# Splitting the attention output: the subtraction moves from the Pool engine to VectorE, and an unrounded copy goes

## The reference, cut to what matters

```
out[chunk] = softmax(q_c @ k_full.T / 8) @ v_full        # 64 keys for 32 queries
x = out as (3072 tokens, 512)
h = x @ w_in                                             # 512 -> 2048
x = (h * sigmoid(h)) @ w_out                             # 2048 -> 512
e = argmax(x @ w_gate + modality_bias[modality_id])      # one of 8 experts
y = gate * (relu(x @ w1[e]) @ w2[e])                     # 512 -> 1024 -> 512
```

## Time and profile before

| | |
|---|---|
| Median of 3 runs | 1037.0 us (1035.72 to 1037.22) |
| The profiled execution, its own time | 1038.32 us |
| Its span, first to last instruction | 1036.7 us |
| TensorE (PE) matmuls busy | 976.9 us, 94% of the span |
| PE weight loads (beside the matmuls) | 843.2 us, 81% |
| ScalarE (ACT) busy | 354.7 us, 34% |
| VectorE (DVE) busy | 309.1 us, 30% |
| Pool engine (POOL) busy | 302.2 us, 29% |
| Mean granted TensorE clock | 0.976 of full speed |

### The profile page before, as it was taken

The page is one execution under the profiler, slowest core; times in us unless marked ns, Lnnn a source line. Parts: engine busy times, 40 slices in busy tenths (PEclk is TensorE's granted clock), DMA queues, the critical chain, the costliest instruction groups (busy, mean ns, idle before and its releaser), DMA issues.

```text
span 1036.7 us, 18125 instructions
## 1 busy us (share of the span) xinstructions
PE 976.9 (94%) x6148; PEld 843.2 (81%) x6149; DVE 309.1 (30%) x749; ACT 354.7 (34%) x728; POOL 302.2 (29%) x318
## 2 busy tenths in 40 slices
PE   4799999999999999999999999993999999999993
PEld 3688888889888888888888989872888888888872
DVE  4421323223232322332333212542532422222221
ACT  4655433343343343343344223330322322222220
POOL 4667122322322222232332232221222222222211
PEclk9899999999999999999999999986999999999997
DMA  7821021421431312242150011320511111111111
GB/s 265 315 79 61 18 76 54 55 77 50 60 73 43 67 45 77 56 53 77 54 55 16 32 42 61 106 38 21 204 44 52 33 41 41 41 41 41 41 42 31
DMA packets 31257, 69.35 MB, mean 67 GB/s; under 512 B 5343, under 2 KB 9439, under 8 KB 31168
## 3 DMA queue, kind: packets, MB, share of 16 engines
q1 hardware_dynamic: 22064, 48.29, 18.0%
q0 software_dynamic: 5904, 13.57, 4.2%
q10 hardware_dynamic: 3200, 6.34, 2.0%
HBM read 55.43 MB, written 13.02 MB: 66 GB/s over the span
## 4 chain that ended last, share of the span: by engine, by line
PE 88%; DMA 6%; issue 1%; DVE 1%; ACT 1%; POOL 1%; SPq 0%; POOLq 0%; ACTq 0%; DVEq 0%
PE bank L1257 26%; PE bank L1243 25%; PE bank L1454 13%; PE bank L1323 13%; DMA token_lists<-token,slot 3%; PE bank L1228 2%; PE bank L1204 2%; DMA q_in<-q_t 2%; PE bank L1465 2%; PE bank L1288 2%; PE bank L1214 1%; PE bank L1312 1%; PE bank L1271 1%; DVE row_sum L884 0%; ACT q_bd L633 0%
## 5 line engine op out<-in xcount | busy, mean ns | idle before, releaser
L558 POOL TENSOR_TENSOR g_lo<-g_raw,g_hi 128x384 fp32r<-128x384 f32 x128 | 131.3, 1026 | 414.6 <-ACT g_hi L767 403.0
L730 ACT ACTIVATE sig<-bank 128x384 f32<-128x384 f32 x128 | 62.8, 491 | 351.2 <-PE bank L1243 351.1
L900 DVE SCALAR_TENSOR_TENSOR g_raw<-sig,bank 128x384 f32<-128x384 f32 x128 | 70.9, 554 | 365.3 <-ACT sig L730 360.1
L1243 PE MATMUL bank<-x_hi,w_hi 128*128 128x384 f32 x512 | 177.4, 346 | 0.1
L1243 PE MATMUL bank<-x_lo,w_hi 128*128 128x384 f32 x512 | 171.7, 335 | 1.5 <-issue 1.5
L1243 PE MATMUL bank<-x_hi,w_lo 128*128 128x384 f32 x512 | 172.8, 338 | 0.0
L1257 PE MATMUL bank<-w_hi,g_hi 128*128 128x512 f32 x384 | 156.7, 408 | 2.1 <-POOL g_lo L558 2.1
L1257 PE MATMUL bank<-w_hi,g_lo 128*128 128x512 f32 x384 | 151.2, 394 | 0.0
L1257 PE MATMUL bank<-w_lo,g_hi 128*128 128x512 f32 x384 | 150.9, 393 | 0.0
L1243 PEld LDWEIGHTS bank<-x_hi,w_hi 128*128 128x128 f32 x512 | 96.3, 188 | 5.6 <-POOL x_lo L482 0.4
L1243 PEld LDWEIGHTS bank<-x_lo,w_hi 128*128 128x128 f32 x512 | 96.4, 188 | 3.2
(11 more groups left out here) (165 smaller groups left out, 1254.4 us busy)
## 6 DMA issues: line engine op xcount, KB each, us to landing
k_in<-k_ctx SPq DMA_DIRECT2D x32, 384.0 KB, 4.4
v_in<-v_ctx SPq DMA_DIRECT2D x32, 384.0 KB, 3.2
w_raw<-w SPq DMA_DIRECT2D x8, 1024.0 KB, 5.3
token_rows<-y_sb ACTq DMA_DIRECT2D x8, 774.0 KB
q_in<-q_t SPq DMA_DIRECT2D x32, 192.0 KB, 3.2
w_raw<-w_in SPq DMA_DIRECT2D x4, 1024.0 KB, 6.9
w_raw<-w_out SPq DMA_DIRECT2D x4, 1024.0 KB, 8.5
list_id<-token_lists POOLq DMA_DIRECT2D x28, 0.5 KB, 2.3
```

The costliest lines, as they stand in the source:

```text
L558: eng.tensor_tensor(g_lo[:, f % 2, :], g_raw[:, f % 2, :], g_hi[:, f % 2, :].bitcast(F32), ALU.subtract).then_inc(g_split, 1)
L730: eng.activation(sig[:, f % 2, :], h_bank[f % 2][:, 0:BLOCK], ACT.Tanh, scale=0.5)\
L900: eng.scalar_tensor_tensor(out=g, in0=s, scalar=1.0, in1=h_bank[f % 2][:, 0:BLOCK], op0=ALU.add, op1=ALU.mult).then_inc(g_done, 1)
L1243: mm = eng.matmul(h_bank[f % 2][:, 0:BLOCK], a, b, start=(k == 0 and n == 0), stop=(k == KC - 1 and n == 2))
```

## The change

The unrounded copy L658, its buffer and Pool's `rest_of_x` go. VectorE gets a `rest_of_x` that subtracts `x_hi` from `o_bank` in PSUM, after `x_hi_done`. In `start()` it stands behind `softmax_out` of the next pair, and for the last pair at the end; in a step it stands at f = 3, 6, 9 and 12 behind `silu(f)`. Since VectorE now reads `o_bank` too, the overwriting waits (`values`, `logits`, `rank`) go by `x_split` in place of `x_hi_done`.

```diff
-        x_raw = early("x_raw", [P, BLOCK])
...
# GpSimd (Pool)
-            def rest_of_x(it, p, par):
-                need(eng, l1_done, (it - 1) * FC)
-                alone(eng, x_hi_done, it * PAIRS + p + 1)
-                eng.tensor_tensor(x_lo[:, par, p, :], x_raw[:, :], x_hi[:, par, p, :].bitcast(F32), ALU.subtract)\
-                   .then_inc(x_split, 1)
...
             def start():
                 for p in range(PAIRS):
-                    if p < PAIRS - 1:
-                        rest_of_first(start_pieces(p))
-                    rest_of_x(0, p, 0)
-                rest_of_first(start_pieces(PAIRS - 1))
+                    rest_of_first(start_pieces(p))
...
-                    if attn and f % 3 == 0 and f >= 3 and f < 3 + 3 * PAIRS:
-                        rest_of_x(it, f // 3 - 1, par)
...
# ScalarE, move_x
-                need(eng, x_split, u)
-                eng.activation(x_raw[:, :], o_bank[:, 0:BLOCK], ACT.Copy)
                 need(eng, l1_done, (it - 1) * FC)
                 eng.activation(x_hi[:, par, p, :], o_bank[:, 0:BLOCK], ACT.Copy).then_inc(x_hi_done, 1)
...
# VectorE
+            def rest_of_x(it, p, par):
+                eng.wait_ge(x_hi_done, it * PAIRS + p + 1)
+                eng.tensor_tensor(x_lo[:, par, p, :], o_bank[:, 0:BLOCK], x_hi[:, par, p, :].bitcast(F32), ALU.subtract)\
+                   .then_inc(x_split, 1)
...
             def start():
                 for p in range(PAIRS):
                     softmax_in(0, p, 0)
                     softmax_out(0, p)
+                    if p > 0:
+                        rest_of_x(0, p - 1, 0)
+                rest_of_x(0, PAIRS - 1, 0)
...
                     if ffn:
                         silu(i, f)
+                    if attn and 1 <= p <= PAIRS and third == 0:
+                        rest_of_x(it, p - 1, par)
...
# TensorE: values, logits, rank
-                need(eng, x_hi_done, u)
+                need(eng, x_split, u)
...
-                need(eng, x_hi_done, it * PAIRS + (t + 1) if attn_now(it) else BLOCKS * PAIRS)
+                need(eng, x_split, it * PAIRS + (t + 1) if attn_now(it) else BLOCKS * PAIRS)
...
-                need(eng, x_hi_done, it * PAIRS + PAIRS if attn_now(it) else BLOCKS * PAIRS)
+                need(eng, x_split, it * PAIRS + PAIRS if attn_now(it) else BLOCKS * PAIRS)
```

## The result

The changed kernel takes 1039.58 us in the median of 11 runs (1038.08 to 1040.93), the kernel before 1037.22 in 11 runs beside it (1034.79 to 1038.15). The ratio is 1.0023, 95% interval 1.0013 to 1.0032: slower by 2.4 us, where no change was forecast. The profiled execution of the changed kernel took 1038.52 us, with a span of 1036.9.

The account below looks back on a forecast made before the run. TensorE was taken as the bound, its matmuls filling 94% of the span. The terms +0.20 and -0.39 sum to -0.19 us, so 1037.0 - 0.2 = 1036.8 us, no change, range 1035.4 to 1038.3.

Parts of the forecast that it names:

- Work that moves: Whole kernel: 32 subtractions leave Pool, 32 copies leave ScalarE, 32 subtractions (17.9 us) come to VectorE; none counts by itself.
- The price of the operation: VectorE's new subtraction with one input in PSUM: 0.56 us each, bounds 0.49 and 0.68; the skill's rule gave 0.53.
- VectorE has the room: Whole kernel: with 309.1 us of work in 1036.7, VectorE can take 17.9 us more.
- Pair 1 to 2, cost 0: Start: the new subtraction delays VectorE's softmax input, but ScalarE's own work holds the exponential; cost 0, cover 0.2 us.
- Pair 2 to 3, +0.20: Start: the same push of 0.56 us makes the next exponential and everything behind it later; +0.20 us, bounds 0 and 0.56.
- The end of the start: Near 37 to 40 us: TensorE's 0.45 us wait goes, but isn't a term; VectorE's later softmax costs 0, cover 0.7 us.
- Step 1, -0.39: Before 55.77 us: the query load sets the time, and without the copy the chain to TensorE is 0.39 us shorter.
- The loop, cost 0: All 28 pairs behind block 0: VectorE's later work stays covered by 1.2 and 6.5 us, so TensorE never waits; cost 0.
- Rival, late clock: Start: TensorE's rise from half to full clock comes about 6.5 us later; +2.3 us, or 1039.3; chance 0.05.
- the 40 that the prediction named as a sign: Start: the forecast is wrong if TensorE's half clock lasts past 40 us.
- Rival, faster by the clock behind the long stall: Near 719 to 726 us: half clock ends some microseconds earlier, up to 3 us of work back, 1034; chance 0.04.
- Rival, VectorE late in the loop: Loop: waiting for x_hi makes silu or the transpose 0.3 us late in 28 pairs; +8.4 us, or 1045; chance 0.03.

Follow-up runs that it names:

- the second profile of the changed kernel: The changed kernel measured once more, unchanged, against the kernel before on the same chip: 1036.97 us, ratio 1.0022.
- the kernel before with 8 memsets: The kernel before with 8 never-executed memsets in VectorE's stream right ahead of the experts: 1034.33 us, ratio 0.9997 to the kernel before.
- the one with the copy put back: The changed kernel with 104 never-executed memsets on VectorE and ScalarE's unrounded copy and its buffer restored, unread: 1033.36 us, ratio 0.9991 to the kernel before.
- the one with all three engines filled: The changed kernel with never-executed instructions added, 104 on VectorE, 31 on ScalarE, 48 on Pool: 1034.05 us, ratio 0.9998 to the kernel before.
- the doubled subtraction: The changed kernel with each new VectorE subtraction done twice and 80 never-executed memsets on VectorE: 1034.21 us, ratio 0.9994 to the kernel before.
- The filled kernels: The changed kernel with never-executed instructions added ahead of the experts on VectorE, in some also on Pool or on Pool and ScalarE: ratios 0.9983 to 0.9998.

## Why the prediction was wrong

The step that failed is **"Work that moves"** with its last sentence, "None of this counts by itself". It counted the executed work of each engine, and that was right. It did not ask where the added instructions put the code behind them. Nor did any rival. The sum and its bounds end at 56 us and the range was built from them and the runs' own spread; who ended the launch, 980 us later, was no part of the sum. The runs showed in its place: 24 more instructions of VectorE's program, executed or not, make its last six branches of L297 or L298 take 13.4 to 13.9 us in place of 4.1, and VectorE then ends 2.1 to 3.2 us behind Pool. The rows were there: L87 of the kernel before shows which engine ends last, and how close the next one is.

Why each branch waits is shown less directly than that the place of the code decides. The fetched pieces come with the waits and go with them; that a loop must lie inside three pieces to stay at hand is an inference from shifts by 8, 24 and 128.

Point by point:

- *The price of the operation*, 0.56: measured 0.557, at most 0.560. Right; the other estimate there, 0.53, was too low.
- *VectorE has the room.* Right for the loop. Its busy time rose by 25.5 us and not by 17.9. L869 took 17.0 us in all, where L884 took 9.9 before, and L873 22.7, where L888 took 20.2; smaller differences of both signs make up the rest. The longer L869 and L873 most likely wait for Pool, which works beside it (argued from the rows, not tried): L869, on 128x6, took 0.58 us at 292.64, while Pool's L545 ran from 292.19 to 293.20; L884 took 0.17 at 291.03, with Pool idle. TensorE waited for none of it.
- *Pair 1 to 2, cost 0.* Right where the three transposes before it take 0.90 us, their time at half clock, as in the profile that the prediction read: from their start to the exponential it is 1.96 us there and in the second profile of the changed kernel. At full clock (0.55) the cover is gone: 1.70 us in the first profile of the changed kernel, where the exponential waits for VectorE, against 1.61 in the kernel before with 8 memsets. That is a cost of 0.09.
- *Pair 2 to 3, +0.20.* Too large, and hidden in this profile by luck. The push on L874 was 0.47 us in place of 0.56, since the new subtraction starts at 24.96, before L873 has ended. ScalarE was busy with `prob_bd` until 27.03, so the exponential, at 27.05, waited for ScalarE itself and not for VectorE, done at 26.77. But ScalarE was that late because the three transposes before it ran at half clock, 0.90 us; in the profile of the kernel before they took 0.55. In two filled forms of the changed kernel (the one with the copy put back and the one with all three engines filled) they took 0.55 too, and there the exponential waited for VectorE and came 0.10 us later behind the transposes than before. So the term is about 0.10 with the transposes at full clock and 0 at half.
- *The end of the start.* Right: no wait of TensorE for `x_lo`, and `x_lo` at 38.16.
- *Step 1, -0.39.* Right where the load binds: 0.36 in the first profile, 0.39 in its own run. The start of step 1's second product moved by -0.27, forecast -0.19, but that number is near by luck: the load released ScalarE 0.09 later here, not 0.20, and between two executions of the kernel before this moved by 2.2 us. In two profiles (all three engines filled, and the doubled subtraction) TensorE didn't wait there at all.
- *The loop, cost 0.* Right: TensorE is busy for 290.0 of 290 us, and the doubled subtraction costs nothing.
- *Rival, late clock:* false, though its 1039.3 us is close to the 1039.58 measured; that is chance. In the changed kernel the clock was back at full at 38.3 us, before at 37.3, and the product at 55.50 was still the earlier one. In the two profiles just named, in which TensorE didn't wait, the half clock lasted to 40.1 and 40.2, past the 40 that the prediction named as a sign, and their times are those of the others.
- *Rival, faster by the clock behind the long stall:* it came in the first profile, which had 5.8 us less of half clock there. But among kernels with the executed work of before the end of the half clock moves by 7.1 us, and the median rose all the same.
- *Rival, VectorE late in the loop:* false by the same rows as the loop.
- *Forecast, 1036.8 and no change:* the moved work alone does that. All changed kernels with the branches put right lie at 0.9983 to 0.9998 of before. With the code where it fell, the closing branches add 3.2 us behind Pool in the first profile and 3.0 in the second, and the kernel is at 1.0023.

In the Trainium skill, "Runtime: NRT & Kernel Launch", section "Instruction fetch mechanics" says that prefetch runs straight ahead and that a taken branch whose target isn't in the current window waits for a fetch. The trace agrees with the second: 2.3 to 3.4 us from the branch to the next instruction at six of the changed kernel's last branches (five of L297, one of L294), where the kernel before has one such, of 2.5 us. The page gives refills of 16 KiB; here the packets of q8 have that size (0.02 MB for one), and those of q14, which come with VectorE's waits, have 8 KiB. The measurement decides.

What stays open: the edit's own gain. In the executions in which the load binds, 0.36 to 0.39 us of it are seen at 55.5 us. The filled kernels gain 0.2 to 1.8 us by their ratios, with intervals that nearly all reach 1.0. Pool's shorter program gives 0.34 us at the end, as shown above. How much is real beyond these, and whether ScalarE's shorter program has a share, isn't settled.

The changed kernel with 104 unexecuted instructions has the lowest ratios here: 0.9983 and 0.999 of the kernel before, and about 0.4% under the change as it was made (1032.96 and 1036.97 us on one chip).

## What to carry to other kernels

An edit that adds instructions to an engine moves every loop and branch behind it, also those that have nothing to do with it. Before a forecast, look at who ends the launch and how late the second engine is. After it, compare the instruction fetches of both kernels in the stretches that the edit doesn't touch. Where a result doesn't fit the work, shift the code alone, with instructions that are never executed, before looking for a cause in the work.

## What the runs showed of the hardware

- A branch of VectorE took 0.2 to 0.3 us to the next instruction when its target was at hand, and 2.1 to 3.7 us when it wasn't (the closing loop and the expert loop of the kernels with slow ones), with fetched pieces of 8192 bytes starting within these waits.
- VectorE's expert loop ran through the four rounds from 800 to 1000 us without any fetch in the kernel before, and with about five pieces in every round after a shift of its code by 8 or 24 instructions. After a shift by 128 it ran without again. The loop's own code is the same in all of them; only its place differs.
- Pool's last instruction, its drain, took 8.72 or 8.73 us in every profile. In the kernel before, Pool ended 14.9 us and VectorE 5.1 us behind the start of VectorE's last product, so VectorE could be 9.8 us later for free. In the changed kernel it took 16.9 us and Pool 13.7, and that went past it by 3.2.
